# Unread products for TensorE in the routing, moved transposes, and all low parts of w1 on VectorE, in an attention and mixture-of-experts kernel

## The chip, the core and the metric

The kernel runs on one core of one Trainium2 chip. The metric is the device time of one execution in microseconds (us). Three executions of the kernel before took 961.91, 962.11 and 962.25 us; the median is 962.11 us.

## What is computed

Three stages follow one another. Attention keeps for each of 2304 queries (4 batches, 8 heads, 576 positions, 64 wide) the 32 largest scores. A dense MLP (512 to 2048 to 512, squared ReLU) takes its result. Then comes a mixture of 8 experts, each 512 to 1024 to 512, in which about half of the rows take part:

```python
skip_score = x @ w_skip
do_compute = skip_score > 0
out = x.copy()
xc = x[do_compute]
logits = xc @ w_gate
e_idx = np.argmax(logits, axis=1)
gate_w = probs[np.arange(len(xc)), e_idx]        # softmax of the logits
for e in range(E):
    mask = e_idx == e
    h = np.maximum(xc[mask] @ w1[e], 0.0)
    y[mask] = gate_w[mask, None] * (h @ w2[e])
out[do_compute] = xc + y
```

## The kernel before

Each engine has its own program, and semaphores with counted increments are all that orders them. In attention VectorE finds the 32 largest of each row (L925, L931), and the dense MLP runs on TensorE in the same time steps, one group of 256 rows behind another (nine groups, `up` L1188 to L1190, `down` L1205 to L1207). A float32 operand is split into a high part (fp32r, made by ScalarE) and a low part (operand minus high part, one subtraction on VectorE or GpSimd), and a product is three products: high by high, low by high, high by low.

**The routing** comes once the last group of the dense MLP is done. ScalarE and VectorE copy its rows out of PSUM (L791, L1017), TensorE transposes them (`transpose_y`, L1220), they are copied again (L799, L1019), and `route` makes logits (L1235). VectorE then picks experts in a chain of small instructions (L953 to L1062), with TensorE called for counts (L1272 to L1277) and for a table of rows (L1282, 18 small products). The chain ends in `gather_tab`, `meta` (which weights each tile of 128 rows uses, and how many tiles there are) and `scatter_tab`. GpSimd gathers the rows of tile s with an indirect DMA (`gather`, L670) and scatters results with another (L692).

**The routed tiles.** These data make 11 tiles, s = 0 to 10. For one tile TensorE does this in order (`routed_tile`, L1296): for each half of the hidden columns three groups of four 128x512 products (L1304 high by high, L1309 low rows by high weights, L1315 high rows by low weights, behind the waits on `w1_low_v` and `w1_low_p`); the four transposes of the rows of tile s + 1 (`transpose_rows`, L1293); for each half four transposes of the hidden values (L1323), behind the wait on `h_done`; and for each half again three groups of four 128x512 products (L1334 high by high, L1339 by the low part of w2, L1342 by `hT_low`).

The other engines work around it, each in a fixed order:
- ScalarE: high parts of w2 (L874: pieces 3, 0, 1), ReLU of half 0 (L892), piece 2, ReLU of half 1 (L895), `hT_high` of both halves (L898, behind `hT_done`), `xT_high` of the next rows (L879), high parts of the next w1 (L868, four pieces).
- VectorE: low parts of w2, pieces 0 to 2 (L1079), `hT_low` of both halves (L1096, one operand in PSUM), `xT_low` of the next rows (L1084, one operand in PSUM), low parts of the next w1, pieces 0 and 1 (L1073), the result `yo` (L1104, behind `down_done`), w1 piece 2.
- GpSimd: low part of w2 piece 3 (L666), low part of the next w1 piece 3 (L660), scatter of the tile (L692, behind `yo`), gather of a later tile (L670).
- SyncE loads the weights of expert e, four transfers of 1 MB each (`load_expert`), into one of two places. From the third expert on it first waits until the splits of the last tile of the expert that held the place are done (L516 to L521).

Before tile 0 VectorE does three pieces of w1 and only then `xT_low`:

```python
            for n in range(3):
                split_w1_low(0, place[0], n)
            split_x_low(0)
```

A piece of weights is 128x1024 float32 throughout. A split has both operands and its result in SBUF.

## Time and profile before

| | |
|---|---|
| median of three executions | 962.11 us |
| the profiled execution | 961.93 us |
| its span, first to last instruction | 960.1 us |
| mean granted TensorE clock | 0.959 of 2.4 GHz |
| busy: TensorE, VectorE, ScalarE, GpSimd | 92%, 89%, 69%, 72% |
| dense MLP's last product starts | 786.7 us |
| tile 0's first product / tile 1's first product | 806.53 / 823.27 us |
| last product group of the last tile starts | 951.96 us |

The span is counted from its first instruction, and 1.83 us of the execution lie around it. In a row of the timeline the first number is the start in us, the second how long it took, then engine, line, operation, output<-inputs, shapes, count, and in brackets the idle time before it and what ended that. Successive instructions of an engine overlap a little, so spacings are read from starts. A matmul's end is modelled. A granted clock of 0.50 is 1.2 GHz, 1.00 is 2.4 GHz.

### The profile page before, as it was taken

To read this page: it belongs to the slowest core of one execution; us is meant where nothing else is said; L and a number is where in the kernel's file an instruction comes from. 1 tells how busy PE (TensorE), PEld (TensorE's weight loads), DVE (VectorE), ACT (ScalarE), POOL (GpSimd) and SP (SyncE) were. 2 spreads that over 40 slices of the span, in tenths; PEclk is the share of its full clock that TensorE was granted. 3 is DMA by queue.
4 is the path that set the end of the run, shared out by engine and by line. 5 is a ranking of instruction groups with operands and counts; after the bars stand their busy time and mean duration, and the time that the engine had idled before them with its cause. 6 is when DMAs were issued, how large, how long until landed. Compare 5 with 4: busy or idle time off the path is not lost.

```text
span 960.1 us, 19356 instructions
## 1 busy us (share of the span) xinstructions
PE 882.6 (92%) x6322; PEld 721.0 (75%) x6322; DVE 854.0 (89%) x1708; ACT 661.8 (69%) x1297; POOL 694.4 (72%) x891
## 2 busy tenths in 40 slices
PE   3566799999999999999999999999999994999996
PEld 1344577888888888888888888888878983777875
DVE  6999999999999998999999999999980237888888
ACT  3677677777787677676778677777764223877875
POOL 2899798877777776787778787778785544566664
PEclk9867699999999999999999999999999995999999
DMA  8964333464354657867436544353343935555970
GB/s 317 376 215 129 118 118 120 157 203 157 115 176 167 192 162 231 241 191 240 136 119 187 169 162 162 127 187 125 132 133 126 333 117 216 200 213 184 337 279 10
DMA packets 69083, 174.76 MB, mean 182 GB/s; under 512 B 20898, under 2 KB 26018, under 8 KB 64624
## 3 DMA queue, kind: packets, MB, share of 16 engines
q1 hardware_dynamic: 67136, 168.39, 52.2%
q0 software_dynamic: 1840, 5.06, 1.6%
q8 instruction: 53, 0.87, 0.4%
q14 instruction: 54, 0.44, 0.2%
HBM read 153.66 MB, written 20.75 MB: 182 GB/s over the span
## 4 chain that ended last, share of the span: by engine, by line
PE 80%; DVE 12%; POOL 2%; issue 2%; ACT 2%; ACTq 0%; DMA 0%; SPq 0%; DVEq 0%; POOLq 0%
PE psum L1188 7%; PE psum L1190 7%; PE psum L1189 7%; PE psum L1128 7%; PE psum L1148 7%; PE psum L1205 7%; PE psum L1206 7%; PE psum L1207 6%; PE psum L1167 6%; DVE top L925 5%; DVE left L931 5%; PE psum L1334 2%; PE psum L1309 2%; PE psum L1131 2%; PE psum L1315 2%
## 5 line engine op out<-in xcount | busy, mean ns | idle before, releaser
L925 DVE MAX8 top<-left 128x8 f32<-128x576 f32 x432 | 305.3, 750 | 0.0
L931 DVE MATCH_REPLACE8 left<-top,left 128x576 f32<-128x576 f32 x288 | 212.1, 745 | 0.0
L565 POOL TENSOR_TENSOR s_sb<-s_sb,below 128x576 f32<-128x576 f32 x144 | 203.3, 1430 | 2.3 <-ACT below L721 2.3
L1188 PE MATMUL psum<-x_high,w_in_high 128*128 128x256 f32 x576 | 169.4, 294 | 1.6 <-POOL x_low L571 1.1
L1190 PE MATMUL psum<-x_high,w_in_low 128*128 128x256 f32 x576 | 163.8, 284 | 0.0
L1189 PE MATMUL psum<-x_low,w_in_high 128*128 128x256 f32 x576 | 163.7, 284 | 0.0
L712 ACT ACTIVATE s_sb<-psum 128x576 f32<-128x576 f32 x144 | 93.5, 650 | 88.6 <-PE psum L1128 72.5
L580 POOL TENSOR_TENSOR square<-relu 128x256 f32<-128x256 f32 x144 | 88.5, 615 | 88.2 <-ACT relu L754 87.7
L1128 PE MATMUL psum<-k_sb,q_sb 64*128 64x288 f32 x512 | 107.2, 499 | 29.6 <-ACT s_sb L712 24.4
L585 POOL TENSOR_TENSOR g_low<-square,g_high 128x256 fp32r<-128x256 f32 x144 | 107.8, 749 | 35.2 <-POOL square L580 27.0
L721 ACT ACTIVATE below<-s_sb,steep_kth 128x576 f32<-128x576 f32 x144 | 110.8, 770 | 29.8 <-POOL neg_max L553 29.8
L1188 PEld LDWEIGHTS psum<-x_high,w_in_high 128*128 128x128 f32 x576 | 110.7, 192 | 5.5 <-POOL x_low L571 1.3
L1205 PE MATMUL psum<-w_ring,g_high 128*128 128x512 f32 x288 | 114.5, 397 | 0.0
L1206 PE MATMUL psum<-w_ring,g_high 128*128 128x512 f32 x288 | 113.7, 395 | 0.0
L1189 PEld LDWEIGHTS psum<-x_low,w_in_high 128*128 128x128 f32 x576 | 110.9, 193 | 3.0
L1207 PE MATMUL psum<-w_ring,g_low 128*128 128x512 f32 x288 | 112.1, 389 | 0.0
L729 ACT ACTIVATE s_sb<-s_sb,neg_max 128x576 f32<-128x576 f32 x144 | 110.8, 770 | 0.0
L1190 PEld LDWEIGHTS psum<-x_high,w_in_low 128*128 128x128 f32 x576 | 110.7, 192 | 0.0
L925 DVE MAX8 top<-s_sb 128x8 f32<-128x576 f32 x144 | 101.3, 746 | 9.4 <-ACT s_sb L712 9.4
L754 ACT ACTIVATE relu<-psum 128x256 f32<-128x256 f32 x144 | 55.5, 385 | 77.7 <-PE psum L1190 75.9
L1148 PE MATMUL psum<-ident,s_sb 128*128 128x128 f32 x576 | 87.2, 297 | 21.4 <-POOL s_sb L559 21.3
L1148 PEld LDWEIGHTS psum<-ident,s_sb 128*128 128x128 f32 x576 | 68.5, 151 | 50.0 <-issue 43.3
(174 smaller groups left out, 1795.3 us busy)
## 6 DMA issues: line engine op xcount, KB each, us to landing
w_ring<-w_split SPq DMA_DIRECT2D x144, 512.0 KB, 4.5
weights<-w SPq DMA_DIRECT2D x32, 1024.0 KB
v_sb<-v_main SPq DMA_DIRECT2D x48, 256.0 KB, 2.6
w_split<-w_ring SPq DMA_DIRECT2D x16, 512.0 KB, 3.8
k_sb<-kT SPq DMA_DIRECT2D x32, 144.0 KB, 4.7
k_sb<-kT SPq DMA_DIRECT2D x32, 128.0 KB, 4.5
q_sb<-qT SPq DMA_DIRECT2D x32, 128.0 KB, 4.3
weights<-w_out SPq DMA_DIRECT2D x1, 4096.0 KB, 13.2
```

Of the source, the lines that this page charges most:

```text
L565: nc.gpsimd.tensor_tensor(s_sb[:, s % SBUFS, n, 0:S], s_sb[:, s % SBUFS, n, 0:S], below[:, n, :], ALU.subtract).then_inc(masked, 1)
L721: nc.scalar.activation(below[:, n, :], s_sb[:, s % SBUFS, n, 0:S], ACT.Relu, bias=steep_kth[:, s % 2, n:n + 1], scale=-STEEP).then_inc(bel ...
L925: v.max(top[:, par, n, r, :], src).then_inc(topk_step, 1)
L931: v.match_replace(left[:, n, :], top[:, par, n, r, :], src, LOWEST).then_inc(topk_step, 1)
L1128: last = t_.matmul(psum[:, n, 0:HALF], q_sb[own, a % RING_A, r * P:(r + 1) * P], k_sb[own, a % RING_A, cols], start=True, stop=True)
L1148: t_.transpose(psum[:, 2 + n, k * P:(k + 1) * P], tiles[:, at:at + P], ident[:, :])
L1188: t_.matmul(dst, wh, x_high[:, j % 2, k, :], start=k == 0, stop=False)
L1189: t_.matmul(dst, wh, x_low[:, j % 2, k, :], start=False, stop=False)
L1190: last = t_.matmul(dst, wl, x_high[:, j % 2, k, :], start=False, stop=k == KC - 1)
L1205: t_.matmul(psum[:, 6 + c, :], gh, wh, start=f == 0, stop=False)
L1206: t_.matmul(psum[:, 6 + c, :], gh, wl, start=False, stop=False)
L1207: last = t_.matmul(psum[:, 6 + c, :], gl, wh, start=False, stop=f == FT - 1)
```

## The change

The new function `keep_busy(n)` issues n products of 128x512 whose result in PSUM bank 4 nobody reads. It is called at six places of TensorE's program: 3 before the last group's transposes, 2 before its logits, 6 before the counts, 16 before the table, 12 after it, 10 before the transposes of tile 0's rows. The transposes of the next tile's rows move from ahead of the hidden values' transposes to between their halves. GpSimd's piece of w1 goes to VectorE (after `yo`), GpSimd's piece of w2 waits for the first half of `hT_high`, and before tile 0 VectorE makes `xT_low` after two pieces of w1 instead of three. ScalarE's order of w1 pieces and the counts in the waits follow from that.

```diff
                     if e >= RING and n == 0:
-                        wait_apart(sp, w1_low_v, 3 * first + 1)
-                        wait_apart(sp, w1_low_p, first + 1)
+                        wait_apart(sp, w1_low_v, 4 * first + 1)
...
-            def split_w1_low(s, at):
-                pool.wait_ge(w1_high_done, 4 * s + 3)
-                raw, high, low = w1_piece(at, 1, 1)
-                nc.gpsimd.tensor_tensor(low, raw, high.bitcast(F32), ALU.subtract).then_inc(w1_low_p, 1)
...
                 pool.wait_ge(w2_high_done, 4 * s + 1)
+                pool.wait_ge(hT_high_done, 2 * s + 1)
                 raw, high, low = w2_piece(at, 3)
...
             gather(1)
-            split_w1_low(0, place[0])
             gather(2)
...
-                split_w1_low(s + 1, place[0])
                 wait(pool, y_stored[x], 16 * (s // DEEP))
...
-                for half, kk in ((0, 0), (0, 1), (1, 1), (1, 0)):
+                for half, kk in ((0, 0), (0, 1), (1, 0), (1, 1)):
...
-                dve.wait_ge(w1_high_done, 4 * s + (1, 2, 4)[n])
-                raw, high, low = w1_piece(at, *((0, 0), (0, 1), (1, 0))[n])
+                dve.wait_ge(w1_high_done, 4 * s + n + 1)
+                raw, high, low = w1_piece(at, n // 2, n % 2)
...
                 split_w1_low(s + 1, place[0], 2)
-
-            for n in range(3):
-                split_w1_low(0, place[0], n)
+                split_w1_low(s + 1, place[0], 3)
+
+            split_w1_low(0, place[0], 0)
+            split_w1_low(0, place[0], 1)
             split_x_low(0)
+            split_w1_low(0, place[0], 2)
+            split_w1_low(0, place[0], 3)
...
+            def keep_busy(n):
+                for _ in range(n):
+                    t_.matmul(psum[:, 4, :], g_high[:, 0, 0:P], g_low[:, 0:2, :].rearrange("p a b -> p (a b)"),
+                              start=True, stop=True)
...
                     if ENDS[j] == t:
+                        if j == GROUPS - 1:
+                            keep_busy(3)
                         transpose_y(j)
                     if ENDS[j] + 1 == t:
+                        if j == GROUPS - 1:
+                            keep_busy(2)
                         route(j)
...
+            keep_busy(6)
             pe.wait_ge(early_sum_set, 1)
             pe.wait_ge(onehot_set, 2)
...
+            keep_busy(16)
             for c in range(NCOL):
                 pe.wait_ge(places_set, 2 if c < EARLY else 3)
...
             last.then_inc(table_done, 1)
+            keep_busy(12)
             pe.wait_ge(meta_set, 2)
...
-                    pe.wait_ge(w1_low_v, 3 * s + 3 + half)
-                    if half == 1:
-                        pe.wait_ge(w1_low_p, s + 2)
+                    pe.wait_ge(w1_low_v, 4 * s + 3 + 2 * half)
...
-                transpose_rows(s + 1)
                 for half in range(2):
+                    if half == 1:
+                        transpose_rows(s + 1)
                     pe.wait_ge(h_done, 2 * s + half + 1)
...
-            for ready in (w1_low_v, w1_low_p, w2_low_v, w2_low_p):
+            for ready in (w1_low_v, w2_low_v, w2_low_p):
                 pe.sem_inc(ready, 1)
+            keep_busy(10)
             transpose_rows(0)
```

## Rows read from the trace of the kernel before

**Rows 1.** Windows of TensorE: busy us (instructions), granted clock, DMA share, GB/s.

```profile
790.00:792.00 2.00, 1.14 (x11) 1.00 1.10 329
792.00:794.00 2.00, 0.30 (x6) 0.62 0.92 365
...
812.00:813.00 1.00, 1.00 (x4) 0.53 0.66 165
813.00:814.00 1.00, 1.00 (x6) 1.00 0.25 99
```

**Rows 2.** Chain of work that ended last (start, us, what), from the routing into tile 0.

```profile
786.86 0.24 PE psum L1207
...
789.18 1.97 PE psum L1235 x16
...
809.64 2.08 PE psum L1309 x4
811.72 1.54 PE psum L1315 x4
813.26 0.93 PE psum L1304 x4
...
815.12 0.91 PE psum L1315 x4
```

**Rows 3.** Timeline from the routing to the first products of tile 0.

```profile
787.87 1.07 PE L1220 MATMUL psum<-ident,rows 128*128 128x128 f32 x8 [0.78 <-ACT rows L791]
...
792.81 0.17 PE L1272 MATMUL psum<-early_sum,ones 128*128 128x8 f16 x1 [1.68 <-DVE onehot L960]
797.38 1.14 PE L1282 MATMUL psum<-values,place_hit 128*128 128x64 f16 x18 [4.26 <-DVE values L1037]
801.35 0.17 DVE L1059 CAST meta<-meta_f 128x13 int32<-128x13 f32 x1
801.94 3.90 ACT L868 ACTIVATE w_high<-weights 128x1024 fp32r x4 [9.94 <-DVE meta L1059]
803.32 2.36 DVE L1073 TENSOR_TENSOR w_low<-weights,w_high 128x1024 fp32r<-128x1024 f32 x2 [1.48 <-ACT w_high L868]
804.72 1.12 PE L1293 MATMUL psum<-ident,tail 128*128 128x128 f32 x4 [6.21 <-DMA tail<-rows_gated,gather_tab]
805.39 2.51 POOL L660 TENSOR_TENSOR w_low<-weights,w_high 128x1024 fp32r<-128x1024 f32 x1
805.88 0.60 ACT L879 ACTIVATE xT_high<-psum 128x512 fp32r<-128x512 f32 x1
805.98 3.01 DVE L1073 TENSOR_TENSOR w_low<-weights,w_high 128x1024 fp32r<-128x1024 f32 x1 [0.30 <-ACT w_high L868]
806.53 2.07 PE L1304 MATMUL psum<-w_high,xT_high 128*128 128x512 f32 x4 [0.69 <-ACT xT_high L879]
808.91 0.68 DVE L1084 TENSOR_TENSOR xT_low<-psum,xT_high 128x512 fp32r<-128x512 f32 x1
```

**Rows 4.** Timeline of tile 1, between its hidden values and its second products.

```profile
828.72 0.60 PE L1293 MATMUL psum<-ident,tail 128*128 128x128 f32 x4
828.92 0.60 ACT L895 ACTIVATE tail<-psum 128x512 f32<-128x512 f32 x1 [0.97 <-PE psum L1315]
829.15 1.07 PE L1323 MATMUL psum<-ident,tail 128*128 128x128 f32 x8
829.79 1.08 ACT L898 ACTIVATE hT_high<-psum 128x512 fp32r<-128x512 f32 x2 [0.28 <-PE psum L1323]
830.76 0.61 ACT L879 ACTIVATE xT_high<-psum 128x512 fp32r<-128x512 f32 x1
```

**Rows 5.** Timeline of tiles 1 and 2: VectorE, GpSimd and the products that wait.

```profile
823.27 1.07 PE L1304 MATMUL psum<-w_high,xT_high 128*128 128x512 f32 x4
...
834.26 1.09 PE L1339 MATMUL psum<-w_low,hT_high 128*128 128x512 f32 x4
834.38 3.34 POOL L660 TENSOR_TENSOR w_low<-weights,w_high 128x1024 fp32r<-128x1024 f32 x1 [4.07 <-ACT w_high L868]
836.12 1.07 PE L1304 MATMUL psum<-w_high,xT_high 128*128 128x512 f32 x4
836.32 0.75 DVE L1104 SCALAR_TENSOR_TENSOR yo<-psum,tail 128x512 f32<-128x512 f32 x1 [0.86 <-PE psum L1342]
836.99 1.82 DVE L1073 TENSOR_TENSOR w_low<-weights,w_high 128x1024 fp32r<-128x1024 f32 x1
...
838.73 3.48 DVE L1079 TENSOR_TENSOR w_low<-weights,w_high 128x1024 fp32r<-128x1024 f32 x3
```

**Rows 6.** Timeline of the last two tiles and the end.

```profile
925.99 1.07 PE L1304 MATMUL psum<-w_high,xT_high 128*128 128x512 f32 x4
...
939.23 1.07 PE L1304 MATMUL psum<-w_high,xT_high 128*128 128x512 f32 x4
...
950.15 4.54 DVE L1073 TENSOR_TENSOR w_low<-weights,w_high 128x1024 fp32r<-128x1024 f32 x2
950.56 3.04 POOL L660 TENSOR_TENSOR w_low<-weights,w_high 128x1024 fp32r<-128x1024 f32 x1 [4.35 <-ACT w_high L868]
...
951.96 1.09 PE L1342 MATMUL psum<-w_high,hT_low 128*128 128x512 f32 x4
954.61 0.74 DVE L1104 SCALAR_TENSOR_TENSOR yo<-psum,tail 128x512 f32<-128x512 f32 x1
```

**Rows 7.** Windows of the last weight transfer: us, granted clock, DMA share, GB/s.

```profile
932.00:934.00 2.00, 1.00 0.30 119
```

More of the change, by code:

```diff
@@ L284, in build @@
         w1_low_v = sem("w1_low_v")
-        w1_low_p = sem("w1_low_p")
         w2_high_done = sem("w2_high_done")
```

## Prediction

> **What bounds the kernel now.** I read the chain of work first, then the windows by granted clock, then the timelines where the chain changes hands. Up to 787.10 us the last product of the dense MLP is on the chain [rows 2]; the diff touches nothing that runs before it, so all of the effect must come from the 173 us behind it. Three stretches follow. In the routing, 787 to 802 us, the chain is VectorE's small instructions with TensorE called in for short jobs [rows 2, 3]. The granted clock there falls from 1.00 to 0.50: the window 792 to 794 shows the mean 0.62, and the clock comes back at about 812.95 (0.53 in the window 812 to 813, 1.00 from then on) [rows 1]. Tile 0, from 806.53 to its last first-stage products at 815.12 + 0.91 = 816.03, is run mostly at the low clock, and between 808.60 (806.53 + 2.07) and 809.64 TensorE also stands: `xT_low` is queued on VectorE behind a third piece of w1 which took 3.01 us [rows 3]. Tiles 1 to 10 are TensorE's own chain at full clock, 12.85 us each from the first product of tile 1 (823.27) to that of tile 2 (836.12), with one stall a tile: the second stage waits for `hT_high` [rows 4, 5]. Last, VectorE is late with the final `yo` [rows 6].
>
> **How VectorE and GpSimd get in each other's way** decides several terms. Three pieces on VectorE alone take 3.48 us, spacing about 1.14 [rows 5]. The piece at 805.98 began inside GpSimd's piece (805.39 to 807.90) and took 3.01 us, about what is left of GpSimd's plus one of its own; the piece at 836.99 took 1.82 us, as GpSimd's ran to 837.72 [rows 3, 5]. So two such subtractions exclude each other. But `yo` at 836.32 lay wholly inside GpSimd's piece and took 0.75 us as everywhere; it has only one operand in SBUF, the other in PSUM, like `hT_low` and `xT_low` [rows 5]. I take it that those two aren't held up either. The Trainium skill, page "SBUF — State Buffer", section "Who interferes with whom", has the same rule: a VectorE instruction with two SBUF inputs and a GpSimd instruction that reads SBUF lock one another out, one with a single SBUF input goes free. It says nothing that would alter the sum; it would fail only if `hT_low` were found waiting.
>
> **The change part by part.**
>
> 1. *Tile 0, -3.98 us.* At the full clock one group of four products takes 0.91 us [rows 2]. The first starts at 806.53, because ScalarE's `xT_high` ends at 806.48 behind its four w1 pieces [rows 3]; I leave that start alone. With `xT_low` before pieces 2 and 3, VectorE has pieces 0 and 1 done at 805.68 [rows 3], does `xT_low` from about 806.55 to 807.2 (0.68 us), and the second group can follow at 807.44 with no stall. Pieces 2 and 3 then end at about 807.2 + 2 x 1.17 = 809.5, before the half-1 group needs them at 811.1. Six groups: 806.53 + 6 x 0.92 = 812.05 instead of 816.03. The bound from below: if the clock is still low, only the reordering counts; the second group starts at 808.4 (four products in 1.88 us at the low clock, from 809.64 to 811.52, the start of the next) rather than 809.64, some 1.3 us.
>
> 2. *The fed products, 0 us.* A 128x512 product of this kind is spaced 0.23 us at the full clock (786.86 to 787.10) [rows 2]. So 3 take 0.7 us (787.1 to 787.8; the transposes began at 787.87), 2 take 0.46 us (the eight transposes' last end, 788.94, lies 0.2 us behind their issue; the logits began at 789.18 [rows 2, 3]), 6 take 1.4 us (791.15 to 792.5; counts at 792.81), 16 take 3.7 us (793.0 to 796.7; table at 797.38), 12 take 2.8 us (798.5 to 801.3; `meta` at 801.52), 10 take 2.3 us (from about 802.2, after its register load, to 804.5; gather lands at 804.72) [rows 3]. Each fits into idle time of TensorE, with 0.7 us to spare for the sixteen but only 0 to 0.3 for the others. For the last, ScalarE is busy until 805.84 (801.94 + 3.90) anyway, so 0.6 us more are free. At the low clock a product costs 0.47 us and sixteen take 7.5 us: that cover would be gone (first rival). Bounds: 0 to +3.2 us. I take 0, since until 787 the clock is at 1.00 and each gap that the feed leaves is under 1 us, except the stretch of transposes and tiny logits products. The ends of the small TensorE jobs are not on the chain where VectorE's own chain is as late, so a faster clock in them gives nothing.
>
> 3. *Transposes between the halves, -0.35 us a tile.* ScalarE starts `hT_high` of half 0 at 829.79, 0.28 us after the ReLU's end at 829.52, because `hT_done` comes late: the rows' four transposes go first. With the hidden values' four first (they need `h_done` of half 0, long there), they end 0.43 us sooner, at about 829.33, and ScalarE can go straight on. Its back-to-back spacing for this shape is 0.485 us (two in 0.97, 829.79 to 830.76) [rows 4], so the start is 828.92 + 0.49 = 829.41, a gain of 0.38; if it waits for the ReLU's end, 829.54, a gain of 0.25. Half 1's transposes waited for that ReLU before too (`h_done` of half 1), and the rows' transposes fill just this wait, so they cost nothing. The next rows' `xT_high` is behind both `hT_high` on ScalarE and isn't late. I take 0.35, as ScalarE's spacing is what other neighbours there show. Eleven tiles: -3.85 us (bounds -2.75 and -4.2).
>
> 4. *The two late tiles, -1.19 us.* Tile 9 takes 939.23 - 925.99 = 13.24 and tile 10 to the end of its products' issue (951.96 + 0.92 = 952.88) 13.65, against 12.85 [rows 5, 6]: 0.39 + 0.80. In both VectorE's pieces meet GpSimd's twice (4.54 us for two in place of 2.3 [rows 6]), and `hT_low` or w1's low part comes late. The change takes GpSimd's w1 piece out and puts its w2 piece where VectorE does `hT_low` and `xT_low`. So these meetings go.
>
> 5. *The last `yo`, -1.53 us.* In tile 2 it starts 0.20 us after the next product could (836.32 against 836.12) [rows 5]; at the end it starts at 954.61, against 952.88 + 0.20 = 953.08. The cause is the 4.54 us pair at 950.15 that waits for GpSimd [rows 6]. What follows `yo` (scatter, its transfer, 1.83 us around the span) stays.
>
> 6. *VectorE's extra piece, GpSimd's wait, the loads: 0 us.* From a tile's first product T: `yo` T+0.2, two w1 pieces to T+3.2 (needed by half 1's low products at T+4.4), three w2 pieces to T+6.6, when `hT_high` is ready at T+6.75; both `hT_low` to T+8.2, `xT_low` to T+8.8. GpSimd starts at about T+6.95, takes 2.5 to 3.34 us [rows 3, 5], and is done at T+9.5 to T+10.3; the low group of half 1 (834.26 less 0.23 for the weight load, less 0.35 gained) needs it at T+10.4. VectorE's next pair waits for GpSimd, then runs T+9.5 to T+11.8; `yo` is due at T+12.7. Behind GpSimd's new wait are queued the scatter and the gather of a later tile; the scatter waits for `yo` anyhow, which comes 3 us later. The margins are 1.2, 1.0, 0.1 to 0.9, and 0.9 us. The loads' first wait now ends at T+3.3 instead of about T+2, their third at T+9.5 instead of about T+7.2; as tiles come 4 to 8 us earlier in all, the last transfer, which is over by 933 [rows 7] with the last tile at 939.2, moves with them and keeps about 4 us. I take 0; the bound on the costly side is 0.5 us a tile, for a GpSimd piece of 3.34 us that also starts behind a piece of VectorE's.
>
> Sum: 3.98 + 3.85 + 1.19 + 1.53 = 10.55. The profiled execution took 961.93, so 951.4; the median was 0.18 above it: **951.6 us**.
>
> **The rivals.**
>
> *The clock falls in spite of the feed* (0.20). For: between 787.9 and 791.1 TensorE has only eight transposes, sixteen products nine columns wide and two fed ones. In the kernel before, that stretch, and 1.4 us of idleness after it, was what preceded the fall [rows 1, 2]. Against: the six fed products stand in that idle time. If it falls at 792.5, the sixteen start slow. In tile 0 the clock came back 3.3 us after TensorE had begun to run without a gap (809.64 to 812.95 [rows 1, 2]); so seven slow ones and nine fast ones, 793.0 + 3.3 + 2.1 = 798.4, +1.1 us at the table; were all slow, +3.2; and tile 0 may lose another 1.6 if its first 3.3 us are slow. I price it at +3.0: 954.6 us. The Trainium skill, page "TensorE: Matmul & The Clock Gate", section "Part 4: PE-mode transpose", speaks for this rival: transposes don't count as activity for the clock gate. The rows can't separate transposes from tiny products here.
>
> *GpSimd's w2 piece is late* (0.10). The margin of 0.1 us in the bad case is thin. With 0.3 us a tile TensorE waits ahead of the second L1339 group: +3.3, 954.9 us.
>
> *VectorE is held by GpSimd's piece in `hT_low`* (0.07), the slower outcome. If GpSimd at T+6.95 gets in first and `hT_low` has to queue, it starts at T+9.5 and ends at T+10.15, while L1342 of half 0 needs it at about T+8.6. That is 1.55 us a tile, eleven tiles: +17, 968.7 us. It decides from 0.96 us a tile on (10.55 / 11). Against it is the `yo` row [rows 5].
>
> *The change doesn't do what it says* (0.07): the clock stays low into tile 0 (term 1 shrinks to 1.3) and `hT_high` doesn't start earlier, as something else on ScalarE is next: 951.6 + 2.7 + 3.85 = 958.1 us, and with a late table up to 961.
>
> **How the numbers follow.** The forecast has 0.56. The low end is the forecast with the larger gain of term 3 and a little of term 4 elsewhere: 950.6. The high end takes in the first two rivals and the smaller gain of term 3: 954.9 + 1.1, so 956.2. Faster by over 0.2% (below 960.2; 0.2% is about what a measurement here can tell from no change): the forecast, the first two rivals and most of the fourth, 0.90, of which I keep 0.88 for what I haven't seen. Within 0.2%: 0.04. Slower: 0.08.
>
> **What would show it.** Windows 790 to 812 with a granted clock of 1.00, and tile 0's first group at 0.92 us (term 1, first rival). The table's products at 797.4 (term 2). `hT_high` without idle time before it, tiles 12.5 us apart, tiles 9 and 10 like the rest (terms 3, 4). `yo` always about 0.75 us and 0.2 us after the products; w1 and w2 pieces on VectorE always about 1.2 us, but for the one behind GpSimd's (terms 5, 6). I am wrong if TensorE waits for GpSimd's `w_low` or VectorE's `hT_low` in every tile, or for a fed product in the routing.

## The result, and the profile after

| | before | after |
|---|---|---|
| median beside each other | 962.03 us (961.91 to 962.25, 4 executions) | 950.79 us (949.67 to 951.14, 4) |
| the profiled execution | 961.93 us | 951.02 us |
| its span | 960.1 us | 949.3 us |
| mean granted TensorE clock | 0.959 | 0.971 |
| dense MLP's last product starts | 786.70 us | 787.05 us |
| tile 0's / tile 1's first product | 806.53 / 823.27 us | 806.75 / 819.30 us |
| last tile's first product | 939.23 us | 931.13 us |
| last product group / last `yo` start | 951.96 / 954.61 us | 942.63 / 943.76 us |

The kernel became faster. The ratio of the times is 0.9881, with a 95% interval from 0.9864 to 0.9898; the medians are 11.2 us apart. The forecast was 951.6 us, so the time came out 0.8 us lower, near the low end of the range (950.6).

Since the diff touches nothing before the dense MLP's last product, I compare from that product to the end of the span. That stretch went from 173.40 to 162.23 us, 11.17 us less. The executions themselves differ by 10.91 us, because the MLP happened to end 0.35 us later. The profiled executions of kernels that are the same up to there differ in that end by up to 1.9 us, so in every comparison of traces below "the rest" is this stretch and not the whole time.

**The clock** answers [rows 1]. Windows of TensorE: the stretch and its length in us, busy us (instructions), granted clock, DMA share, GB/s.

```profile
790.00:792.00 2.00, 2.00 (x17) 1.00 1.01 340
792.00:794.00 2.00, 1.82 (x14) 1.00 1.02 376
808.00:812.00 4.00, 4.00 (x19) 1.00 0.39 122
```

At 792 to 794 it was 0.62; now it is 1.00, and it stays there until 948.7 us.

**The routing and tile 0** answer [rows 3]. Timeline: start, duration, engine, line, operation, output<-inputs, shapes, count, idle time before and what ended it. The lines that were L1207, L1220, L1235, L1282, L1293, L1304, L1309, L1315 and L1323 of TensorE are now L1201, L1214, L1229, L1289, L1301, L1312, L1317, L1321 and L1330; L1237 is the fed products.

```profile
791.35 1.65 PE L1237 MATMUL psum<-g_low,g_high 128*128 128x512 f32 x6
...
793.33 3.90 PE L1237 MATMUL psum<-g_low,g_high 128*128 128x512 f32 x16
...
797.75 0.96 PE L1289 MATMUL psum<-values,place_hit 128*128 128x64 f16 x18 [0.53 <-DVE values L1029]
...
803.11 2.52 PE L1237 MATMUL psum<-g_low,g_high 128*128 128x512 f32 x10 [1.59 <-issue]
...
805.47 0.60 PE L1301 MATMUL psum<-ident,tail 128*128 128x128 f32 x4
...
806.75 1.19 PE L1312 MATMUL psum<-w_high,xT_high 128*128 128x512 f32 x4 [0.69 <-ACT xT_high L871]
807.78 1.08 PE L1317 MATMUL psum<-w_high,xT_low 128*128 128x512 f32 x4
...
812.33 0.60 PE L1330 MATMUL psum<-ident,tail 128*128 128x128 f32 x4
```

From 793.33 on the sixteen stand, and they leave 0.53 us of idle time ahead of the table, so they don't delay it. Ahead of the last ten TensorE stands for 1.59 us. The rows' transposes stand right behind the ten, and no wait for the gather shows. Tile 0's products follow one another without a stall, and the hidden values' transposes start 5.58 us after its first product (806.75 to 812.33) instead of 9.34 us (to 815.87).

**Tile 1 and the start of tile 2** answer [rows 4, 5]. `hT_high` is now L890, `hT_low` L1087, `yo` L1095, the w2 pieces L1070 on VectorE and L660 on GpSimd, the second products L1341, L1346 and L1349.

```profile
823.84 1.07 PE L1321 MATMUL psum<-w_low,xT_high 128*128 128x512 f32 x4
824.75 0.60 PE L1330 MATMUL psum<-ident,tail 128*128 128x128 f32 x4
824.95 0.60 ACT L887 ACTIVATE tail<-psum 128x512 f32<-128x512 f32 x1 [0.97 <-PE psum L1321]
825.44 0.59 ACT L890 ACTIVATE hT_high<-psum 128x512 fp32r<-128x512 f32 x1
...
826.09 1.20 PE L1341 MATMUL psum<-w_high,hT_high 128*128 128x512 f32 x4
826.28 2.41 POOL L660 TENSOR_TENSOR w_low<-weights,w_high 128x1024 fp32r<-128x1024 f32 x1 [1.77 <-ACT hT_high L890]
...
826.92 0.69 DVE L1087 TENSOR_TENSOR hT_low<-psum,hT_high 128x512 fp32r<-128x512 f32 x1 [0.16 <-ACT hT_high L890]
827.53 0.68 DVE L1075 TENSOR_TENSOR xT_low<-psum,xT_high 128x512 fp32r<-128x512 f32 x1
...
829.87 1.09 PE L1346 MATMUL psum<-w_low,hT_high 128*128 128x512 f32 x4
...
831.73 1.07 PE L1312 MATMUL psum<-w_high,xT_high 128*128 128x512 f32 x4
```

ScalarE starts `hT_high` 0.49 us after the ReLU and no longer waits for TensorE; from the third group of half 1 to the second products it is 2.25 us (823.84 to 826.09), 0.38 less than before. VectorE's `hT_low` and `xT_low` lie wholly inside GpSimd's piece (826.28 to 828.69) and take 0.69 and 0.68 us, as they do alone. GpSimd is done 1.18 us before its product group needs the piece (829.87). A tile takes 12.42 or 12.43 us, all of them, the last ones too.

**The end** answers [rows 6].

```profile
942.63 1.09 PE L1349 MATMUL psum<-w_high,hT_low 128*128 128x512 f32 x4
943.76 0.75 DVE L1095 SCALAR_TENSOR_TENSOR yo<-psum,tail 128x512 f32<-128x512 f32 x1 [1.01 <-PE psum L1349]
...
945.38 1.14 POOL L684 DMA_INDIRECT out<-yo,scatter_tab  x1 [4.84 <-DVE yo L1095]
```

`yo` starts 0.21 us after the point at which a next product could (942.63 + 0.92).

The account of the rest, stretch by stretch, before minus after: tile 0's start 0.13 (19.83 and 19.70 us behind the MLP's last product), tile 0 4.19 (16.74 and 12.55), tiles 1 to 8 3.32 (102.72 and 99.40), tile 9 0.81 (13.24 and 12.43), tile 10 1.23 (13.65 and 12.42), the last `yo` 1.52 (1.73 and 0.21), and from there to the end -0.03. The sum is 11.17.

### The profile page after: what moved, and what is told of

It reads as the page before. It is cut to its first block, busy times and chain, and to the rows that moved or that the text cites. A ratio compares the mean times of both kernels' runs of the same rounds, so it can differ in the third digit from the quotient of the medians.

```text
span 949.3 us, 19452 instructions
## 1 busy us (share of the span) xinstructions
PE 886.7 (93%) x6371; PEld 727.2 (77%) x6371; DVE 848.1 (89%) x1720; ACT 661.8 (70%) x1297; POOL 658.6 (69%) x879
## 4 chain that ended last, share of the span: by engine, by line
PE 83%; DVE 11%; POOL 2%; ACT 1%; issue 1%; DMA 0%; ACTq 0%; SPq 0%; POOLq 0%; DVEq 0%
PE psum L1182 7%; PE psum L1184 7%; PE psum L1183 7%; PE psum L1122 7%; PE psum L1142 7%; PE psum L1199 7%; PE psum L1200 7%; PE psum L1201 7%; PE psum L1161 6%; DVE top L917 5%; DVE left L923 5%; PE psum L1341 2%; PE psum L1346 2%; PE psum L1349 2%; PE psum L1312 2%; PE psum L1321 2%
## 5 line engine op out<-in xcount | busy, mean ns | idle before, releaser
L1201 PE MATMUL psum<-w_ring,g_low 128*128 128x512 f32 x288 | 112.1, 389 | 0.0
```

The source lines that it names most:

```text
L1201: last = t_.matmul(psum[:, 6 + c, :], gl, wh, start=False, stop=f == FT - 1)
```

## The experiments

The theory was that of the prediction: an unbroken clock and the order of `xT_low` for tile 0; ScalarE's earlier `hT_high` in every tile; VectorE's and GpSimd's pieces kept apart at the end. After the result three things were open: whether the feed matters by itself, which part of the moved splits carries the late tiles and what keeps the others at 12.42, and what sets the start of tile 0. "Rest" below is the stretch from the MLP's last product to the span's end, in each kernel's profiled execution: 173.40 before, 162.23 after. The medians of the kernel before beside them were 961.62 us (first four runs), 962.59 (the next four), 962.0 (e9 to e11), 962.1 (e12) and 961.24 (e13 and e14).

**e1: the changed kernel again.** No edit.

> The changed kernel once more, beside the three that follow, on the same chip. All theories: 950.8 us against 962.0 of the kernel before. Its executions spread over 1.5 us (949.67 to 951.14), those of the kernel before over 0.3. If that spread comes from the clock of TensorE in the routing or tile 0, fast and slow executions will show different granted clocks; if it is chance of this chip, the spread may be gone here.

950.83 us (949.05 to 951.42), ratio 0.988 [0.9864, 0.9897], rest 162.55. It tells what two profiled executions of one kernel differ by in the rest: 0.3 us, all of it at tile 0's start (20.01 against 19.70). The clock in the routing and in tile 0 is 1.00 in both, so the spread of the executions doesn't come from there; the last section says where some of it lies.

**e2: everything but the feed.**

```diff
             def keep_busy(n):
-                for _ in range(n):
+                for _ in range(0):
```

> The changed kernel without the 49 unread products. Theory 1 (they hold TensorE's clock, and that is worth part of tile 0's gain): the clock falls near 792 us and comes back about 3.3 us after tile 0's first product; the six groups of tile 0's first stage then take some 7.3 us instead of 5.6: 952.5 us. Rival (the reordering of the low parts made the whole gain of tile 0, the clock was coming back anyway): 950.8 us. Rival (all of the gain was the clock's): 954.5 us.

952.27 us, ratio 0.9901 [0.9885, 0.9918], rest 164.94. Windows of TensorE and, below, tile 0's timeline:

```profile
790.00:792.00 2.00, 0.31 (x6) 0.56 1.05 369
808.00:810.00 2.00, 2.00 (x6) 0.50 0.15 60
810.00:811.00 1.00, 1.00 (x4) 0.63 0.00 0
```

```profile
804.90 2.07 PE L1312 MATMUL psum<-w_high,xT_high 128*128 128x512 f32 x4 [1.36 <-ACT xT_high L871]
...
806.77 1.91 PE L1317 MATMUL psum<-w_high,xT_low 128*128 128x512 f32 x4
...
810.19 1.35 PE L1312 MATMUL psum<-w_high,xT_high 128*128 128x512 f32 x4
```

The clock falls at 790.3 and comes back at 810.7, 5.8 us into tile 0, which takes 15.33 us instead of 12.55. All that is lost lies in that tile: the low clock in the routing delays nothing (tile 0 starts 19.67 us behind the MLP). In the rest the feed is worth 2.4 to 2.7 us by this execution and the two of the changed kernel. That is the upper part of what it is worth: in e4 below, the same code up to there lost only some 1.3 us in tile 0 (14.30, less the 0.42 of the transposes, against 12.55), and the medians of e1 and e2 differ by 1.44. The 952.5 us expected were met by luck: tile 0 lost 2.8 us and not 1.7, and the MLP had ended 1.3 to 1.8 us sooner than in the changed kernel's two executions.

**e3: the transposes alone,** in the kernel before.

```diff
-                transpose_rows(s + 1)
                 for half in range(2):
+                    if half == 1:
+                        transpose_rows(s + 1)
```

> The kernel before with the moved transposes alone. Theory 1 (the parts add up): 11 tiles by 0.43 us, -4.7 us: 957.3 us. Rival (it needs the new division of the low parts): VectorE's three w2 pieces take 5.68 us in every second tile and hT_low then starts at T+8.05, about when L1342 needs it; the 0.43 us are lost to that wait there and kept in the others: about -2.4 us, 959.6 us, with TensorE waiting for hT_low.

957.41 us, ratio 0.9957 [0.9941, 0.9974], rest 168.67, so 4.73 less. Tiles take 12.42 or 12.43 us where VectorE is not late; tiles 3 and 9 take 12.61 and tile 10 13.01, where TensorE waits 0.32 us for `hT_low`, and the last `yo` starts at 949.70, 1.74 after the products, behind two pieces of w1 that took 4.54. So the change's 0.42 us a tile is there, and nothing is gained at the last `yo`. Tiles 9 and 10 are still late, but they gain 0.63 and 0.64 us, 0.2 more each than the others.

**e4: the splits alone.** The changed kernel without the feed (as e2) and with the rows' transposes back in front (e3's edit undone).

> The changed kernel without the unread products and with the transposes back in front: the new division of the low parts and the early xT_low alone. Theory 1: -1.2 us for tiles 9 and 10, -1.5 for the last yo, -1.9 for tile 0 (no stall before its second group, at the low clock): 957.4 us, tiles 12.85 us apart. Rival (the new division slows the other tiles, hidden in the changed kernel by the moved transposes): tiles more than 12.85 us apart, over 959 us.

956.69 us, ratio 0.9946 [0.9929, 0.9962], rest 168.28. Every tile takes 12.85, the ninth and the tenth too, and the last `yo` starts 0.21 us after its products. Tile 0 takes 14.30 us, as the clock comes back 2.9 us into it (808.4), sooner than in e2. Both kernels are the same up to there, so this moment varies from one execution to the next, and with it the price of a fall. (Here tile 0 still has the transposes in front, which costs it the 0.42 us that e2's is spared.)

**e5: the feed alone,** in the kernel before: the six calls of `keep_busy`.

> The kernel before with the 49 unread products alone. Theory 1: the clock stays at full speed through the routing, but xT_low still queues behind VectorE's third w1 piece, so TensorE stands from about T0+0.9 to T0+3.1 in tile 0, and then runs five groups at 0.91 us: tile 0 takes 14.9 us instead of 16.7, all later tiles 12.85: 1.9 us faster, 960.0 us. Rival (the clock was all of tile 0's gain): tile 0 takes 13 us.

960.6 us, ratio 0.9978 [0.9966, 0.9991], ten executions; rest 174.81 us, which is 1.41 more than before. Timeline of tile 0 and windows of TensorE (the line numbers are those of before, moved by the new function):

```profile
805.26 1.19 PE L1318 MATMUL psum<-w_high,xT_high 128*128 128x512 f32 x4 [0.69 <-ACT xT_high L879]
...
808.23 2.07 PE L1323 MATMUL psum<-w_high,xT_low 128*128 128x512 f32 x4 [1.78 <-DVE xT_low L1084]
```

```profile
806.00:807.00 1.00, 0.45 (x2) 1.00 0.00 0
807.00:808.00 1.00, 0.00 (x0) 0.73 0.00 0
808.00:809.00 1.00, 0.77 (x2) 0.50 0.00 0
```

The feed carries the clock through the whole routing, and then it falls in the stall behind `xT_low` and stays low until 814.3. Tile 0 takes 17.86 us. But the profiled execution is one of the slowest two of the ten (958.64 to 961.77), and the median is 2.0 us below that of the kernel before beside it, close to the 960.0 expected. Three executions took 958.64 to 958.72, 3 us less than the profiled one, which is more than the end of the MLP moves (1.9 us, and here it was early, at 785.19). So in those three the rest must have been shorter than in the kernel before, and tile 0 can't have lost what it lost here; there is no trace of them. Alone the feed can gain about 2 us, and with the stall behind it that gain is not safe.

**e6: only the late feed.** The calls with 3, 2 and 6 are dropped; 16, 12 and 10 stay.

```diff
-                        if j == GROUPS - 1:
-                            keep_busy(3)
...
-                        if j == GROUPS - 1:
-                            keep_busy(2)
...
-            keep_busy(6)
```

> The changed kernel without the first three calls (3, 2 and 6 products); the 16, 12 and 10 stay. Theory 1 (the early eleven keep the clock up, and a feed at the low clock delays the table): the clock falls near 791 us, the sixteen products take 5.4 to 7.5 us instead of 3.7, the table's products start 1.1 to 3.2 us later than in the changed kernel (10.7 us after the dense MLP's last product there), tile 0's first product too, and tile 0 itself runs at the full clock: 952 to 954 us. Rival (the later feeds are enough): no difference, 950.8 us.

950.95 us, ratio 0.9889 [0.9865, 0.9913], rest 163.64:

```profile
790.00:791.00 1.00, 0.00 (x0) 0.67 1.18 299
```

```profile
791.50 6.54 PE L1237 MATMUL psum<-g_low,g_high 128*128 128x512 f32 x16
...
797.88 0.70 PE L1284 MATMUL psum<-values,place_hit 128*128 128x64 f16 x18
```

The clock falls at 790.3, the sixteen take 6.54 us instead of 3.90, and the table is late (12.65 us behind the MLP instead of 10.70); tile 0 starts 21.34 us behind the MLP, 1.3 to 1.6 later than in the two executions of the changed kernel. But the clock is back at 797.2, and tile 0 takes 12.56. So in this execution the first eleven fed products protect the table, not tile 0. It is also the nearest measure of the first rival: 1.3 to 1.6 us at tile 0's start and nothing in tile 0. The median, 950.95, is within 0.2 us of the changed kernel's, against 952 to 954 expected, so the loss rests on one trace; in that execution the MLP ended 1.3 to 1.8 us sooner (785.23), which hides it in the whole time.

**e7: GpSimd's wait taken out** of the changed kernel.

```diff
-                pool.wait_ge(hT_high_done, 2 * s + 1)
```

> The changed kernel with GpSimd's w2 piece no longer behind the first half of hT_high. Theory 1 (the wait keeps two subtractions apart): GpSimd does the piece while VectorE has its three w2 pieces, VectorE loses some 2.4 us there in most tiles, hT_low starts near T+9 while TensorE wants it at T+8.6, tiles take 12.8 to 13.3 us instead of 12.43: 954 to 960 us. Rival (VectorE has the slack): tiles 12.43 us apart, 950.8 us.

960.93 us, ratio 0.9983 [0.9972, 0.9994], rest 172.52: nearly the whole gain is gone. Timeline of tile 1:

```profile
822.78 5.68 DVE L1069 TENSOR_TENSOR w_low<-weights,w_high 128x1024 fp32r<-128x1024 f32 x3
...
824.85 2.52 POOL L659 TENSOR_TENSOR w_low<-weights,w_high 128x1024 fp32r<-128x1024 f32 x1
...
828.38 1.27 DVE L1086 TENSOR_TENSOR hT_low<-psum,hT_high 128x512 fp32r<-128x512 f32 x2
...
829.11 1.19 PE L1348 MATMUL psum<-w_high,hT_low 128*128 128x512 f32 x4 [0.55 <-DVE hT_low L1086]
```

Without the wait GpSimd does its piece amid VectorE's three, which take 5.68 us instead of 3.49 (the sum of both engines' work, nearly), and `hT_low` queues behind them. All tiles take 13.25 to 13.29. The wait is worth 0.84 us a tile here, where VectorE has all of w1. It doesn't make anything earlier by itself; it moves the piece to where VectorE's instructions have one operand in PSUM.

**e8: 32 fed products ahead of the table** instead of 16.

```diff
-            keep_busy(16)
+            keep_busy(32)
```

> The changed kernel with 32 unread products instead of 16 before the table. Theory 1 (these products are ahead of the table in TensorE's queue and the cover ends 0.5 us behind the sixteen): 32 take 7.4 us, the table's products start 3.1 to 3.2 us later, all behind it too: 953.9 us. Rival (the clock gains more than the delay): below 953 us.

952.89 us, ratio 0.9908 [0.9884, 0.9932], rest 164.88. The 32 take 7.53 us, the table comes right behind them, 2.93 us later behind the MLP than in the changed kernel (13.63 against 10.70), and tile 0 starts 22.32 behind the MLP: 2.3 to 2.6 us later than in the two executions of the changed kernel. The sixteen more take 3.6 us; what is past their cover delays the table, and most of that delay reaches tile 0. No clock is gained for it.

**e9: `xT_low` back behind the third piece of w1** in the changed kernel.

```diff
-            split_x_low(0)
             split_w1_low(0, place[0], 2)
+            split_x_low(0)
```

> The changed kernel with xT_low of tile 0 after three w1 pieces, as in the kernel before, but with GpSimd's piece gone. Theory 1 (what held xT_low was GpSimd's piece in the middle, not the order): the third piece takes 1.2 us and ends at T0+0.5, xT_low at T0+1.2, TensorE's second group 0.2 to 0.4 us later than in the changed kernel: tile 0 takes 12.8 to 12.9 us instead of 12.55, 951.1 us. Rival (the order itself is worth the 1.3 us of my bound): tile 0 takes 13.8 us, 952.1 us.

949.51 us, ratio 0.9868 [0.9847, 0.989]. Three executions took 949.13 to 949.6 us, so no more than the changed kernel's. The profiled one took 953.13. In it the first three pieces are done in 3.50 us, by 806.17, before `xT_high` was there, and `xT_low` starts at 807.18, right behind it. In this execution the gather was late, so the trace doesn't show what the order costs when the rows are in time: the third piece ended 20.26 us behind the MLP, and the second group of tile 0 would then come some 0.3 us late, an estimate from the spacings here. By the three other executions the order alone is worth at most some tenths of a us. In the kernel before it was GpSimd's piece that made VectorE's third last 3.01 us [rows 3] instead of about 1.2, and that piece is gone. The profiled execution also shows the clock fall behind a complete feed (TensorE's timeline):

```profile
805.86 0.66 PE L1301 MATMUL psum<-ident,tail 128*128 128x128 f32 x4 [1.17 <-DMA tail<-rows_gated,gather_tab]
807.20 1.35 PE L1312 MATMUL psum<-w_high,xT_high 128*128 128x512 f32 x4 [0.69 <-ACT xT_high L871]
...
808.35 1.91 PE L1317 MATMUL psum<-w_high,xT_low 128*128 128x512 f32 x4
```

The gather landed late, 6.1 us after its issue instead of the 4.7 of e1, TensorE idled 1.17 and 0.69 us around four transposes, the clock was low from 808.1 to 811.5, and tile 0 took 14.18 us.

**e10: GpSimd keeps its piece of w1,** with feed, transposes, GpSimd's wait and the early `xT_low` (added to the kernel before). It asks whether moving that piece to VectorE was needed.

```diff
                 pool.wait_ge(w2_high_done, 4 * s + 1)
+                pool.wait_ge(hT_high_done, 2 * s + 1)
...
-            for n in range(3):
-                split_w1_low(0, place[0], n)
+            split_w1_low(0, place[0], 0)
+            split_w1_low(0, place[0], 1)
             split_x_low(0)
+            split_w1_low(0, place[0], 2)
```

> The changed kernel with the last w1 piece back on GpSimd, behind its w2 piece, which keeps its wait; everything else as changed. Theory 1 (after hT_high two pieces on GpSimd, 5 us, and two on VectorE, 2.3 us, exclude each other, and end at about T+14.3): VectorE or GpSimd is late for yo or for half 1 of the next tile, tiles take 12.8 to 13.5 us instead of 12.43: 955 to 962 us. Rival (the wait alone does it, the w1 piece could have stayed): tiles 12.43 us apart, 951 us.

951.83 us, ratio 0.9892 [0.9868, 0.9916], rest 164.11. Tiles take 12.42 to 12.47 and tile 0 12.55: for them the move was not needed. The end:

```profile
941.19 2.75 POOL L660 TENSOR_TENSOR w_low<-weights,w_high 128x1024 fp32r<-128x1024 f32 x1 [1.71 <-ACT w_high L869]
944.34 1.54 POOL L693 DMA_INDIRECT out<-yo,scatter_tab  x1 [0.41 <-issue]
```

In the last tile `yo` is in time, but GpSimd still has its piece (up to 943.94) and the last scatter follows it. From the start of `yo` to the span's end it is 6.87 us, 1.35 more than after (5.52).

**e11: the rows of tile 0 earlier.** `xT_high` ahead of ScalarE's fourth w1 piece, `gather_tab` ahead of one reduction in VectorE's chain, and 6 instead of 10 fed products at the end.

```diff
-            split_w1_high(0, *place)
+            split_w1_high(0, *place, pieces=((0, 0), (0, 1), (1, 0)))
...
+            raw, high, _ = w1_piece(place[0], 1, 1)
+            nc.scalar.activation(high, raw, ACT.Copy).then_inc(w1_high_done, 1)
...
-            keep_busy(10)
+            keep_busy(6)
```

> A further step on the changed kernel: xT_high of tile 0 comes ahead of ScalarE's fourth w1 piece, gather_tab ahead of a 0.4 us reduction on VectorE, and 6 unread products instead of 10 before tile 0's transposes. Theory 1 (ScalarE's four pieces and the gather both end within 0.1 us of each other and set tile 0's start): tile 0's first product comes 19.1 to 19.4 us after the dense MLP's last instead of 19.7 to 20.0; 950.1 to 950.5 us, which is less than the spread between executions. Rival (the six products are too few and the clock falls): tile 0 takes over 13.5 us, 952 us.

950.27 us, ratio 0.988 [0.9856, 0.9903], rest 162.62: no gain. Tile 0 starts 20.00 behind the MLP, as it did. The timeline of SyncE's queue, VectorE and GpSimd shows why:

```profile
787.34 2.05 SPq L425 DMA_DIRECT2D weights<-w  x2
...
791.85 0.38 SPq L431 DMA_DIRECT2D rows_gated<-gate  x1
...
796.92 0.19 DVE L1038 TENSOR_SCALAR gather_tab<-psum 128x32 uint32<-128x32 f32 x1
...
799.08 1.24 POOL L664 DMA_INDIRECT tail<-rows_gated,gather_tab  x1 [15.69 <-issue]
```

`gather_tab` is there at 797.11, but GpSimd issues the gather at 799.08. It also waits for the small store of the gates (4 KB), which was issued behind two loads of 1 MB and took 5.9 us to land (797.75). The same store landed after 4.5 to 5.3 us in the five kernels whose routing has no feed (before, e2, e3, e4, e12), and there the gather is issued 1.42 or 1.43 us after the start of `gather_tab`, so `gather_tab` holds it. In all with a feed and this order of the loads the store took 5.7 to 6.0 us, and where the table isn't late the gather is issued 1.53 to 1.84 us after the start of `gather_tab` (2.16 here, where `gather_tab` comes sooner). So the feed comes with a store about 1 us slower, which costs the gather 0.1 to 0.4 us in the changed kernel; why, no run shows. Then the gather itself has 4.75 us from its issue to the transposes (803.83), and TensorE waits for it.

**e12: GpSimd's wait alone,** one line added to the kernel before.

```diff
                 pool.wait_ge(w2_high_done, 4 * s + 1)
+                pool.wait_ge(hT_high_done, 2 * s + 1)
```

> The kernel before with one line more: GpSimd's w2 piece waits for the first half of hT_high. Its w1 piece stays on GpSimd, nothing is fed, no transpose is moved. Theory (the wait alone ends the two late tiles): tiles 1 to 10 all 12.85 us, the last yo 0.2 us after the products could go on instead of 1.7, but GpSimd is then still busy with a w1 piece for a tile that doesn't come and scatters 1.3 to 1.4 us late: 2.7 us won in TensorE's and VectorE's part, 1.35 lost behind it, 960.6 us. Rival (the late tiles came from the w1 piece): tiles 9 and 10 still take 13.2 and 13.6 us, 962 us.

960.19 us, ratio 0.9981 [0.9971, 0.9991], rest 171.65, 1.75 less than before. Tiles 1 to 10 take 12.84 or 12.85, the last two of them too, and the last `yo` starts 1.12 us after the last group's start instead of 2.65. But GpSimd's w1 piece now runs 948.63 to 951.73, the last scatter comes behind it, and from `yo` to the span's end it is 6.57 us instead of 5.49. So the wait ends the late tiles and the late `yo`; the moved w1 piece is what keeps the scatter from paying for it.

**e13 and e14: what holds the gather of tile 0.** e13 is e11 with the store of the gates ahead of all four loads of 1 MB instead of between them. e14 is e13, and then SyncE waits until the gather of tile 0 has landed before it issues the loads.

```diff
-                    if e == 1 and n == 2:
+                    if e == 1 and n == 0:
...
+                        sp.wait_ge(gathered[0], 16)
```

> The kernel of the third step again, with one condition of SyncE's program changed: the store of the last gates (4 KB) is queued ahead of expert 1's first two loads instead of between its halves. Theory 1 (GpSimd's first gather waits for that store, which takes 5.7 to 5.9 us under the two 1 MB loads, and not for gather_tab): the store lands in 2 to 3 us, the first gather is issued 0.7 to 1.7 us earlier, tile 0's first product comes 18.8 to 19.4 us after the dense MLP's last instead of 20.0, 949.6 us. Rival (the gather takes longer under loads that are then still running): no gain, 950.3 us.

> As the one before, and SyncE also waits for tile 0's gather before it loads expert 1. Theory 1 (both transfers are slow because the loads keep the DMA engines full, share 0.94 to 1.06 from 790 to 804): the gather lands in 2.5 to 3.5 us instead of 4.5 to 6, tile 0's first product comes 18.5 to 19.2 us after the dense MLP's last and 0.5 us more evenly; the load of expert 1 is over near 815 us and still in time: 949.3 us. Rival (expert 1 comes too late, ScalarE waits for it in tile 1): tile 1 takes over 13 us, 951 us or more.

e13: 953.39 us (950.43 to 955.5, the widest spread here), ratio 0.991 [0.988, 0.994], rest 164.37. e14: 948.96 us (948.65 to 950.41), ratio 0.9869 [0.985, 0.9889], rest 161.58. SyncE's queue, GpSimd and the transposes of tile 0's rows, first of e13, then of e14:

```profile
793.41 0.36 SPq L431 DMA_DIRECT2D rows_gated<-gate  x1
...
793.81 9.15 SPq L425 DMA_DIRECT2D weights<-w  x4
...
799.86 1.20 POOL L664 DMA_INDIRECT tail<-rows_gated,gather_tab  x1 [14.97 <-issue]
...
807.14 0.66 PE L1303 MATMUL psum<-ident,tail 128*128 128x128 f32 x4 [2.74 <-DMA tail<-rows_gated,gather_tab]
```

```profile
792.18 0.36 SPq L431 DMA_DIRECT2D rows_gated<-gate  x1
...
798.62 1.20 POOL L665 DMA_INDIRECT tail<-rows_gated,gather_tab  x1 [14.97 <-issue]
...
802.12 0.82 SPq L425 DMA_DIRECT2D weights<-w  x2
...
803.00 0.60 PE L1304 MATMUL psum<-ident,tail 128*128 128x128 f32 x4
...
804.29 1.19 PE L1315 MATMUL psum<-w_high,xT_high 128*128 128x512 f32 x4 [0.69 <-ACT xT_high L872]
```

In both the gather is issued 13.18 us behind the MLP's last product, 0.73 sooner than in e11, so the store is out of the way. The store waits for the gates, so in e13 the loads queued behind it start late too, 7.13 us behind the MLP instead of 2.17, and all four run beside the gather. The gathered rows are there 7.28 us after the issue, and tile 0 starts 21.80 us behind the MLP. In e14 the gather lands 3.5 us after its issue (SyncE's loads wait for it and start at 802.12), the transposes don't wait, and tile 0 starts at 18.85, the earliest of all (it then takes 12.70, 0.15 more than after). Against e11 the gather is done 2 us sooner: 0.73 by the earlier issue, and 1.2 by the shorter transfer (3.5 instead of 4.7 us). Only 1.15 of it shows, as ScalarE's three pieces of w1 (up to 803.72) are next in setting tile 0's start. Between e13 and e14 the loads beside the gather are the only difference. But with two loads beside it the gather took anything from 3.6 (e2, e6, e8) to 6.1 us (e9), so what holding them back saves varies. e14 is the fastest version that was run. Its median is 1.8 us below the changed kernel's, but the intervals of the two ratios overlap, and the rest is only 0.65 to 0.97 us shorter than in the two executions of the changed kernel; the remaining difference of the profiled executions lies before the routing, where e14's was 1.1 to 1.6 us ahead.

## Where the prediction was right, and the step that failed

The mechanism was the one forecast in its main parts: sum 10.55, measured 11.17 in the stretch that the diff touches. The step that failed is the third, the size of the moved transposes' gain: put at 0.35 us a tile with 4.2 us in all as its bound, it measured 0.42 us a tile and 4.6 us in all. The median of 950.79 still lies in the range, 0.2 us above its low end. With the 0.35 us by which the MLP ended later in the profiled execution and 0.11 less around the span, that is the 10.91 between the two profiled executions, within rounding.

1. *Tile 0, predicted -3.98, measured -3.76.* Up to the hidden values' transposes; the start was left alone and moved by 0.13. Of the 0.22 that are missing 0.16 lie in the reading: 816.03 is a modelled end, and what follows the last group starts at 815.87. The two halves of the step, clock and order, can't be added: with the splits but no feed tile 0 takes 14.30 or 15.33 us (e4, e2), as the clock comes back at different times, and with the feed alone the clock can be lost again in the stall (e5). The lower bound of 1.3 was for the order with a low clock. The reason given for the order was only half right. Of the 1.8 us by which the third piece was too long, all came from GpSimd's piece running against it; the place of `xT_low` behind that third is itself worth at most some tenths (e9). Either edit is enough: with GpSimd's piece kept and `xT_low` early tile 0 takes 12.55 us too (e10).

2. *The fed products, 0.* Right in size: the table isn't late and `meta` isn't. The last ten do delay the transposes, which stand right behind them, but ScalarE is busy with w1 until 806.2 anyway, as the step said. Two things in the step were not so. It said that every gap left is under 1 us, but ahead of the last ten TensorE stands for 1.59 us; the clock held all the same. And it had no term for the small store, which is slower with the feed and holds the gather back by 0.1 to 0.4 us in the two executions of the changed kernel (e11); in one of them `xT_high` waited 0.21 us for the transposes (e1). The cover ends where it was put: 16 more cost 2.3 to 2.6 us (e8), and at the low clock the sixteen take 6.54 (e6).

3. *Transposes between the halves, predicted -0.35 a tile and -3.85 in all: the step that failed, by its size.* Measured -0.42 a tile, over eleven tiles -4.6. ScalarE's start moved by 0.38 exactly, its own spacing of 0.49 behind the ReLU; I had taken 0.35 between that and waiting for the ReLU's end. The rest, 0.04, is in the second stage, which went from 5.68 to 5.64 us a tile; TensorE waits for nothing there before or after, and what makes it shorter stays open. e3 has the same 0.42 in the kernel before, so it is this edit. That is 0.75 us more than forecast and more than the bound of -4.2. With tile 0's 0.22 less and its start's 0.13 more it makes the 0.62 us by which the sum was short; what is left of the 0.8 is no more than executions differ by.

4. *The two late tiles, predicted -1.19, measured -1.20.* Right in size (0.81 + 1.23, less two times 0.42). The cause is GpSimd's wait, not the moved piece of w1: e12 has it with the wait alone, and e10 without the move. The share isn't exact, since the transposes alone already give 1.27 us on these two tiles (e3) and the wait alone 1.21 (e12), together more than the 2.04 measured.

5. *The last `yo`, predicted -1.53, measured -1.52.* Right, and here the two edits share the work. The wait makes `yo` punctual (e12, e10), and the moved w1 piece keeps the scatter free, worth 1.35 us (e10). The step said that what follows `yo` stays; it does only because of the move.

6. *VectorE's extra piece, GpSimd's wait, the loads, 0.* Right in the changed kernel; the w2 piece took 2.41 us, a little under the 2.5 to 3.34 that was allowed. What the step did not see is how much hangs on the wait: once w1 has left GpSimd, its absence would cost 0.84 us in every tile (e7). I had priced only what the wait could cost.

**The rivals.** The fall of the clock in spite of the feed didn't happen in the routing of any kernel with the whole feed. It did in tile 0, of e9 once and of e5. Its price when it falls early was 1.3 to 1.6 us in the one trace there is (e6), all of it from the late table, below the 3.0 given. The lateness of GpSimd's piece: refuted, 1.18 us of margin. VectorE held in `hT_low`: refuted by 0.69 us inside GpSimd's piece. The Trainium skill, page "SBUF — State Buffer", section "Who interferes with whom", states this rule, and the traces here agree both ways: 0.69 us for the instruction with one operand in PSUM, and 5.68 instead of 3.49 us for three with both in SBUF (e7). "The change doesn't do what it says": refuted.

As to transposes and the clock, what preceded the fall in e2 was eight transposes, sixteen products nine columns wide and idle time. The Trainium skill, page "TensorE: Matmul & The Clock Gate", section "Part 4: PE-mode transpose", says that a transpose doesn't engage the full clock level, since it doesn't count as busy time of TensorE in the same way. In the changed kernel the same instructions stood with five and six fed products around them and the clock held; no run here separates transposes from narrow products.

## What to carry to other kernels

Where two engines exclude each other, don't ask how to share the work but beside what each piece lies: a wait placed on purpose moved GpSimd's piece beside instructions with a PSUM operand and was worth 0.84 us a tile here, with no work saved. What unread products gain can be lost again in a stall that follows them before the dense work, and they are free only up to the idle time that covers them; read both from the timeline before adding them. And when a start doesn't move though its engine's chain got shorter, look at the small transfers behind big ones. Queuing the store first alone made tile 0 later in the trace there is (21.80 against 20.00 us behind the MLP), because the loads then ran beside the gather; with 4 MB of loads that nobody needed yet held back as well it came 1.15 us sooner than in e11.

## What was unexpected of the hardware

- **When the clock comes back is not fixed.** It came back 2.9 us (e4) and 5.8 us (e2) after tile 0's first product, in code that is the same up to there, and 6.4 us after it in the kernel before, where TensorE stood in between [rows 1, 3]. Tile 0 took 14.30, 15.33 and 16.74 us.
- **Nor does the length of a gap tell whether it falls.** TensorE stood 2.74 us and, after 0.66 us of transposes, 0.69 more in e13, and the windows up to 812 us show 1.00. It fell after 1.17 and 0.69 us around the same transposes in e9, and within 1.78 us of idle time in e5. I have no reading of the traces that sorts the three.
- **A small transfer behind large ones is slow:** 4 KB took 4.5 to 6.0 us to land behind two loads of 1 MB (4.6 before, 5.7 after), and 2.5 to 3.0 us ahead of them (e13, e14). It took 4.5 to 5.3 without the feed and 5.7 to 6.0 with it, for a reason that no run shows. The gather of tile 0 landed 3.6 to 6.1 us after its issue beside two loads, 7.2 beside four (e13), and 3.5 with the loads held back (e14).
- **The dense MLP's end moved by up to 1.9 us** between executions that are the same up to there (785.12 to 787.05 us). It came latest where the clock had reached full level for good latest: at 110.9 us in the first case, at 122.7 in the other. The ten profiled executions in which that was before 113 us have the end at 785.12 to 785.91, and the five in which it was at 116 to 117 us at 786.50 to 786.70. In the medians this is noise as large as some of the effects above, which is why they are read from the rest.
